# Attention scores of a float32 kernel: the two high-high products of a pair of key chunks as two 64-row matmuls on the halves of TensorE's array

## The reference

```python
scores = (1/S) * z @ z.T            # z: (2, 3008, 64)
attn   = np.maximum(scores, 0) ** 2
x      = u * (attn @ v)             # u, v: (2, 3008, 256)
```

## Time and profile before

| | before |
|---|---|
| time, median of 3 runs | 1649.8 us (1649.75 to 1649.91) |
| span of the profiled execution, first to last instruction | 1648.0 us |
| its own time beside the span | the median stands 1.8 us above the span; no other time was taken of it |
| PE (TensorE matmul) busy | 1638.2 us, 99%, 7176 matmuls |
| PEld (weight loads) busy | 1353.7 us, 82%, 7176 loads |
| DVE busy | 857.0 us, 52% |
| ACT busy | 742.0 us, 45% |
| granted TensorE clock | 1.000 |
| phase A on TensorE | 5.47 to 531 us |

### The profile page before, as it was taken

One profiled execution on the slowest core, in us unless ns is written; L12 is line 12 of the kernel. 1 busy time (PEld: TensorE's weight loads), 2 busy tenths in 40 slices (PEclk: granted clock), 3 DMA queues, 4 the chain that ended last, 5 costly groups with the idle time before them and its releaser, 6 DMA issues.

```text
span 1648.0 us, 19288 instructions
## 1 busy us (share of the span) xinstructions
PE 1638.2 (99%) x7176; PEld 1353.7 (82%) x7176; DVE 857.0 (52%) x885; ACT 742.0 (45%) x886; POOL 0.2 (0%) x4
## 2 busy tenths in 40 slices
PE   8999999999999999999999999999999999999999
PEld 6888888888888888888888888888888888888887
DVE  8766678766667544444444444543333333333332
ACT  7555567555556444444444444533333333333332
POOL 0000000000000000000000000000000000000000
PEclk9999999999999999999999999999999999999999
DMA  4100013200002100000000000210000000000000
GB/s 127 45 25 25 25 44 96 70 26 25 35 19 78 62 26 25 25 25 25 25 25 25 25 16 22 92 35 23 25 25 25 13 24 12 25 25 25 12 13 13
DMA packets 18605, 55.76 MB, mean 34 GB/s; under 512 B 2064, under 2 KB 2320, under 8 KB 18576
## 3 DMA queue, kind: packets, MB, share of 16 engines
q1 hardware_dynamic: 18576, 55.37, 10.2%
HBM read 36.86 MB, written 18.51 MB: 34 GB/s over the span
## 4 chain that ended last, share of the span: by engine, by line
PE 99%; DVE 1%; DMA 0%; ACT 0%; issue 0%; DVEq 0%; ACTq 0%
PE acc L276 17%; PE acc L275 17%; PE acc L274 17%; PE hidden L274 13%; PE hidden L276 13%; PE hidden L275 13%; PE hidden L294 4%; PE hidden L295 4%; PE acc L333 0%; PE acc L334 0%; DVE part_lo L441 0%; DMA stage<-zT 0%; DVE region_z L441 0%; DVE full L475 0%; ACT first L396 0%; DVE region_vl L441 0%
## 5 line engine op out<-in xcount | busy, mean ns | idle before, releaser
L441 DVE TENSOR_TENSOR part_lo<-full,part_hi 128x1004 fp32r<-128x1004 f32 (+1 forms) x384 | 381.2, 993 | 418.9 <-ACT part_hi L412 159.3
L274 PE MATMUL acc<-part_hi,region_vh 128*128 128x502 f32 x648 | 252.3, 389 | 1.1 <-DVE part_lo L441 1.1
L276 PE MATMUL acc<-part_hi,region_vl 128*128 128x502 f32 x648 | 253.3, 391 | 0.0
L275 PE MATMUL acc<-part_lo,region_vh 128*128 128x502 f32 x648 | 252.9, 390 | 0.0
L410 ACT ACTIVATE part_hi<-first 128x1004 fp32r<-128x1004 f32 x144 | 150.3, 1044 | 209.7 <-PE acc L276 196.2
L481 DVE TENSOR_TENSOR full<-hidden,first 128x502 f32<-128x502 f32 x144 | 98.1, 681 | 246.3 <-ACT first L404 246.3
L404 ACT ACTIVATE first<-hidden 128x502 f32<-128x502 f32 x144 | 85.1, 591 | 266.8 <-PE hidden L276 266.8
L412 ACT ACTIVATE part_hi<-full 128x1004 fp32r<-128x1004 f32 x96 | 100.3, 1045 | 169.7 <-PE acc L276 164.4
L475 DVE TENSOR_TENSOR full<-first 128x1004 f32<-128x1004 f32 x144 | 172.7, 1199 | 1.4 <-ACT first L396 1.0
L478 DVE TENSOR_TENSOR full<-hidden,first 128x1004 f32<-128x1004 f32 x96 | 115.6, 1204 | 111.0 <-ACT first L400 111.0
L400 ACT ACTIVATE first<-hidden 128x1004 f32<-128x1004 f32 x96 | 96.9, 1009 | 129.9 <-PE hidden L276 129.9
(11 more groups left out here) (66 smaller groups left out, 2521.0 us busy)
## 6 DMA issues: line engine op xcount, KB each, us to landing
xs<-x_out SPq DMA_DIRECT2D x24, 502.0 KB, 3.1
x_in<-xs SPq DMA_DIRECT2D x24, 502.0 KB, 3.5
stage<-vP SPq DMA_DIRECT2D x24, 256.0 KB, 2.6
u_in<-uT SPq DMA_DIRECT2D x12, 502.0 KB, 4.0
yT<-x_out SPq DMA_DIRECT2D x11, 502.0 KB, 2.7
stage<-w SPq DMA_DIRECT2D x12, 384.0 KB, 3.0
stage<-w SPq DMA_DIRECT2D x8, 512.0 KB, 3.6
stage<-zT SPq DMA_DIRECT2D x12, 256.0 KB, 2.6
```

What stands on the lines that cost most here:

```text
L274: pe.matmul(dst, hi, mov_hi, start=start, stop=False)
L275: pe.matmul(dst, hi, mov_lo, start=False, stop=False)
L276: return pe.matmul(dst, lo, mov_hi, start=False, stop=stop)
L441: return ve.tensor_tensor(dst, whole, hi.bitcast(F32), ALU.subtract)
```

## The change

For each step of phase A the four full matmuls of `H` are replaced by two full ones and two on 64 rows. The full ones are the mixed products of the two chunks, and come first. Then follow the high-high product of the first chunk, which takes keys and tokens from rows 0 to 63 of `z_hl`, and that of the second chunk, from rows 64 to 127 of `z_lh`, where the high part stands also. They write the same two banks as before. The low-low product is computed no longer. And TensorE's program (PE alone) writes out all 12 tiles of phase A one after the other instead of looping over tiles 1 to 4 and 7 to 10; ACT, DVE and SP keep their loops, and their instructions are the same.

```diff
-def tile_runs():
+def tile_runs(unrolled):
+    for T in range(unrolled):
+        yield T, T, False
     for a, b in ((0, TPB), (TPB, NT), (NT, 2 * NT), (2 * NT, 3 * NT)):
+        if a < unrolled:
+            continue
         yield a, a, False
         yield a + 1, b - 2, True
         yield b - 1, b - 1, False
...
                     tokens = bass.ds((T - b * TPB) * TOK, TOK)
+                    keys = [slice((2 * p + c) * P, (2 * p + c + 1) * P) for c in range(2)]
+                    dst = [hidden[:, bank + c, 0:TOK] for c in range(2)]
                     for c in range(2):
-                        keys = slice((2 * p + c) * P, (2 * p + c + 1) * P)
-                        dst = hidden[:, bank + c, 0:TOK]
-                        pe.matmul(dst, z_hl[b][:, keys], z_hl[b][:, tokens], start=True, stop=False)
-                        last = pe.matmul(dst, z_hl[b][:, keys], z_lh[b][:, tokens],
-                                         start=False, stop=True)
+                        pe.matmul(dst[c], z_hl[b][:, keys[c]], z_lh[b][:, tokens],
+                                  start=True, stop=False)
+                    pe.matmul(dst[0], z_hl[b][0:DQK, keys[0]], z_hl[b][0:DQK, tokens],
+                              start=False, stop=True)
+                    last = pe.matmul(dst[1], z_lh[b][DQK:P, keys[1]], z_lh[b][DQK:P, tokens],
+                                     start=False, stop=True)
...
-            over_tiles(pe, tile)
+            over_tiles(pe, tile, unrolled=NT)
```

More of the change, by code:

```diff
@@ L105, in tile_runs, with over_tiles @@
         yield b - 1, b - 1, False
-def over_tiles(eng, body):
-    for a, b, looped in tile_runs():
+def over_tiles(eng, body, unrolled=0):
+    for a, b, looped in tile_runs(unrolled):
         if looped:
```

## The result

The changed kernel takes 1674.21 us (median of 4 runs, 1673.19 to 1674.42) against 1649.86 us, a ratio of 1.0147 with a 95% interval of 1.0133 to 1.0161: 24.4 us slower. The span of its profiled execution is 1672.4 us, 24.4 us more too.

What follows compares the result with a forecast made beforehand. PE bounds the kernel, at 227 ns per matmul. Gains of 15.4 us (tiles 1 to 11) and 0.5 us (tile 0) bring the span from 1648.0 to 1632.1, plus 1.8 gives 1633.9 us; range 1616 to 1667.

Steps and rivals of the forecast that it cites:

- What bounds the kernel: Whole kernel: PE, busy 99%, sets the time as number of matmuls times their distance of 227 ns.
- Room for a faster PE: Phase A: DVE and ACT have slack, 1.9 us for `part_lo`; only tile 0 is tight, losing half its gain.
- my sum: Phase A: 15.4 us gained in tiles 1 to 11 plus 0.5 us in tile 0, together 15.9 us.
- Step 2, side by side: Half products of each phase A step: the second starts 110 ns late, pair costs 337 ns, gain 117 ns (bounds 0 to 227).
- Step 3, the switches: Two changes a step between full array and halves, before the halves and at `O`: taken as nothing, or small.
- the third rival: Every phase A step: the array empties at each switch, exposing 163 ns tails and perhaps loads; 1665, 1680 or 1696 us; 0.32.
- The threshold: Phase A switches: emptying decides the result from 112 ns a switch with full overlap, 59 ns if halves start 110 ns apart.
- The rule on step 3: Phase A switches: the skill says changing tiling mode drains TensorE; the earlier trace, having no switch, could not confirm it.
- Step 5, loops: PE's phase A program: removing loops is worth nothing; fetching the longer program priced at 0 to 1 us.
- the rival that came true: The third rival: the array empties at every switch of phase A, slower by 15, 30 or 47 us; chance 0.32.
- its sign: Phase A tile length of 44.6 to 47.3 us, expected in the profile if the array empties at switches.

Runs made afterwards that it cites:

- experiment 2: The changed kernel with the second chunk's high-high product also taken from rows 0 to 63, so both halves use the same rows: 1706.57 us.
- the groups: The changed kernel with the scores of two or three steps in one piece, one pair of switches per piece: 1653.51 and 1643.64 us.
- groups of three: The changed kernel with scores of three steps in one piece: 1643.64 us; with tile 0 as in the kernel before, 1637.54 us.
- experiments 2 and 9: Experiment 2 and, as number 9, the changed kernel without the first chunk's high-high product, one half between the switches: 1673.88 us.
- experiment 3: The changed kernel in the order mixed, half, mixed, half: four switches a step, no halves side by side: 1763.63 us.
- experiment 4: The changed kernel with the mixed products split too, three pairs of 64-row products a step, still two switches: 1673.49 us.
- experiment 1: The kernel before with only TensorE's program for phase A written out over all 12 tiles: 1649.79 us against 1649.87.

## Why the prediction was wrong

It said 1633.9 us, 1616 to 1667, faster at 0.60. It is 1674.2, slower.

- *What bounds the kernel, and that a matmul costs its distance of 227 ns*: right. The distances inside `O` are the same after, and experiment 2 shows the same distance for halves run in turn.
- *Room for a faster PE*: not tested by the change itself, but by the groups. In tiles 1 to 11 DVE and ACT kept up (with groups of three PE waited 0.2 us for them there). In tile 0 they did not: there the order of the waits mattered, more than the busy share that I had read. The clock had no term in my sum: in tile 0 the full clock came at 15.0 us instead of 9.9, which cost about 1 us.
- *Step 2, side by side*: the direction right, the middle value wrong. I had let the second load start with the first half's matmul, 110 ns late, because loads are issued one ahead in the earlier trace rows. Both loads go out together (107.03), and the gain is the full 227 ns (experiments 2 and 9). Rows with one kind of matmul said nothing of loads for two separate halves.
- *Step 3, the switches*: this is the step that failed: "I take nothing, or small: the results of a matmul still in flight go to another bank, which is the case between any two chunks now". A different bank was no reason; nothing in the trace tied the switch to PSUM. A switch costs 198 ns. It has both parts that the third rival listed, but the tail is shorter. I had priced it at the 163 ns by which a matmul's row outlasts the distance; the wait of the load beyond the distance is 83 ns (experiment 3). The load's 110 ns are as in the earlier trace rows. The threshold was right: 112 ns a switch if halves overlap fully. The 197.5 ns of experiment 3 are above it, and 144 x (2 x 197.5 - 227) = 24.2 us, against 24.4 measured.
- *The rule on step 3*: that changing the tiling mode, not just the tile, drains TensorE (the Trainium skill, TensorEngine Tiling (Array Packing), Key Properties). The trace agrees: 198 ns each way, the new matmul starting when the row of the last is just over (0.42 against 0.39 us), and from half to half no cost is seen (experiment 4). That the array is empty in between no row shows. That matmuls on different row groups start some 4 ns apart (the Trainium skill, TensorE: Matmul & The Clock Gate, The mechanism) agrees as well: 107.03 and 107.04, and 3 to 4 ns in each of the 144 pairs. Both rules held together, and I had set one against the other.
- *Step 5, loops*: right, 0 (experiment 1).
- *The range*: the rival that came true, with 0.32 of the chances, was split into 15, 30 and 47 us, and the range ended between the first two. A price with two parts that may each be exposed or not has values between the sums, and 24 us was one of them. The tile's length of 45.3 us lies between the 44.6 and 47.3 that were to be its sign.

## What to carry to other kernels

A gain that needs another mode of an engine is to be weighed per switch, not per instruction: here a switch between the full array and its halves costs 0.87 of a 502-column matmul, so each pair of switches needs at least two pairs of halves between them before it pays, and the more the better. Group the work of one mode as far as buffers allow (scores of three steps turned 24 us of loss into 12 us of gain), but leave the start of a pipeline, where other engines are the bound, in its finest order. When matmul busy time stays at 99% and the time grows, read the weight loads and the distance of starts: the emptied array shows as a busy one.

## What the runs showed of the hardware that was not expected

- The weights of the new mode are not loaded beside the start of the last matmul of the old mode, as they are between matmuls of one kind: the load goes out 0.31 to 0.32 us after that matmul's start, in both directions, and 0.10 to 0.11 us more pass before its matmul begins. With 502 columns a switch costs 198 ns (396 to 405 ns a pair in three kernels). How it depends on the columns wasn't tried.
- Halves at the start of the kernel go with a later full clock. The four kernels whose first scores are full matmuls have it on record from 8.9 to 11.7 us, the seven whose first scores hold halves from 14.4 to 21.9 us. In experiment 4 the first 18 products are all halves with no switch between them, and the full clock came at 14.5 us. What holds it back no run tells.
- Two weight loads for different halves of the array go out within 10 ns of each other and cost nothing beside each other, though full loads in the earlier trace rows are 0.23 us apart. A load of 64 rows lasts 0.18 us and a full one 0.19 us.
- A pair of 64-row matmuls of 502 columns takes as long as one full matmul, and one alone takes as long as the pair (1673.88 against 1674.21 us).
